# Attention and mixture of experts on one core: scores as three products of split q and k, the parts made by GpSimd

## The reference

```python
scores = scale * np.matmul(q, k.transpose(0, 1, 3, 2))
scores = np.where(mask, scores + bias[None], -1000000000.0)   # mask: 0 <= row - key < 128
attn = softmax(scores)
x = matmul(attn, v)                                            # (2304, 512)
expert = argmax(x @ w_gate); gate = its softmax probability
h = np.maximum(disp[e] @ w1[e], 0); y = h @ w2[e]               # disp: the rows of expert e, up to capacity
out[row] = gate * y[row]
```

## Time and profile before

| | |
|---|---|
| median of 3 runs | 436.08 us (435.88 to 436.37) |
| profiled execution | 436.13 us |
| its span, first to last instruction | 434.4 us |
| mean granted TensorE clock | 0.993 of full speed |
| TensorE matmul busy | 418.4 us (96%), 2860 instructions |
| VectorE busy | 276.9 us (64%) |
| ScalarE busy | 217.9 us (50%) |
| GpSimd busy | 100.0 us (23%) |

### The profile page before, as it was taken

The page is one execution under the profiler, slowest core; times in us unless marked ns, Lnnn a source line. Parts: engine busy times, 40 slices in busy tenths (PEclk is TensorE's granted clock), DMA queues, the critical chain, the costliest instruction groups (busy, mean ns, idle before and its releaser), DMA issues.

```text
span 434.4 us, 11059 instructions
## 1 busy us (share of the span) xinstructions
PE 418.4 (96%) x2860; PEld 341.3 (79%) x2861; DVE 276.9 (64%) x829; ACT 217.9 (50%) x576; POOL 100.0 (23%) x154
## 2 busy tenths in 40 slices
PE   6999999999999999899999999999999999999982
PEld 5778788787878877688888888888888888888871
DVE  4887788798988967865656627634657676233220
ACT  3878787787877743455544405515444445111100
POOL 5092066001301202412222211222222111222201
PEclk9999999999999999999999999999999999999997
DMA  9999399269621111465666605641676652111100
GB/s 175 238 272 197 81 285 222 80 212 246 152 74 50 51 39 24 154 230 192 204 237 223 230 27 166 212 148 61 212 238 207 208 193 94 48 48 38 45 27 16
DMA packets 78861, 63.59 MB, mean 146 GB/s; under 512 B 61614, under 2 KB 61614, under 8 KB 78832
## 3 DMA queue, kind: packets, MB, share of 16 engines
q1 hardware_dynamic: 71504, 51.66, 42.7%
q0 software_dynamic: 3520, 10.76, 7.6%
q10 hardware_dynamic: 3808, 0.80, 1.1%
HBM read 53.77 MB, written 10.23 MB: 147 GB/s over the span
## 4 chain that ended last, share of the span: by engine, by line
PE 90%; DVE 6%; issue 1%; DMA 1%; ACT 0%; POOL 0%; DVEq 0%; POOLq 0%; SPq 0%
PE ps L1282 52%; PE ps L1158 8%; PE ps L1126 7%; PE ps L1139 6%; PE ps L1170 5%; PE ps L1104 4%; PE ps L1302 4%; PE ps L1275 2%; DVE probs L760 1%; DMA q_rows<-in_q 1%; DVE weights_sb L1029 1%; DVE kT L772 1%; DVE sums_eps L778 0%; PE ps L1194 0%; DVE probsT L325 0%
## 5 line engine op out<-in xcount | busy, mean ns | idle before, releaser
L1282 PE MATMUL ps<-weights_sb,rowsT_hi 128*128 (+1 forms) x336 | 107.8, 402 | 1.3 <-DVE rowsT_lo L1016 1.3
L1282 PE MATMUL ps<-weights_sb,hiddenT_hi 128*128 x320 | 98.7, 389 | 1.2 <-DVE hiddenT_lo L1009 1.2
L698 ACT ACTIVATE hidden<-ps 128x512 f32<-128x512 f32 x20 | 11.9, 598 | 141.9 <-PE ps L1282 141.9
L1029 DVE TENSOR_TENSOR weights_sb<-raw,weights_sb 128x1024 f32 (+1 forms) x56 | 67.2, 1221 | 15.5 <-issue 10.0
L602 ACT ACTIVATE probs<-probs,mins 128x256 f32<-128x256 f32 (+2 forms) x160 | 73.8, 467 | 0.0
L1282 PEld LDWEIGHTS ps<-weights_sb,rowsT_hi 128*128 128x128 f32 x336 | 61.1, 188 | 15.2 <-issue 1.9
L1282 PEld LDWEIGHTS ps<-weights_sb,hiddenT_hi 128*128 128x128 f32 x320 | 60.0, 188 | 14.1 <-issue 1.4
L1282 PE MATMUL ps<-weights_sb,rowsT_lo 128*128 (+1 forms) x168 | 66.2, 394 | 0.0
L1009 DVE TENSOR_TENSOR hiddenT_lo<-ps,hiddenT_hi 128x512 fp32r<-128x512 f32 x40 | 25.8, 686 | 58.1 <-ACT hiddenT_hi L702 58.1
L1282 PE MATMUL ps<-weights_sb,hiddenT_lo 128*128 x160 | 62.4, 390 | 0.0
L687 ACT ACTIVATE weights_sb<-raw 128x1024 f32 (+1 forms) x56 | 56.6, 1068 | 0.0
(11 more groups left out here) (152 smaller groups left out, 535.6 us busy)
## 6 DMA issues: line engine op xcount, KB each, us to landing
raw<-in_moe_w SPq DMA_DIRECT2D x64, 512.0 KB, 4.4
q_rows<-in_q SPq DMA_DIRECT2D x16, 256.0 KB, 5.8
v_rows<-in_v SPq DMA_DIRECT2D x16, 256.0 KB, 4.5
x_rows<-x_sb SPq DMA_DIRECT2D x16, 256.0 KB, 4.6
k_rows<-in_k SPq DMA_DIRECT2D x13, 256.0 KB, 5.5
k_rows<-in_k ACTq DMA_DIRECT2D x3, 256.0 KB, 5.7
q_rows<-in_q SPq DMA_DIRECT2D x4, 128.0 KB, 3.9
k_rows<-in_k SPq DMA_DIRECT2D x4, 128.0 KB, 4.3
```

What stands on the lines that cost most here:

```text
L1029: vec.tensor_tensor(weights_sb[:, slot, 2 * layer + 1, part].rearrange("p s n -> p (s n)"), raw[:, j, :], weights_sb[:, slot, 2 * layer, p ...
L1282: ins = te.matmul(dst, left[a], right[c], start=first and n == 0, stop=last and n == 2)
```

## The change

ScalarE and VectorE write turned q and k no longer to `qT` and `kT` but back over the tile's own places in `q_rows` and `k_rows`, in float32. GpSimd makes of them the parts `qT` (hi and lo, two tiles deep), `kT_hi` and `kT_lo` in float32r: for q one copy and one subtraction of 512 elements, for k one copy of 512 and four subtractions of 128, for each of the tiles 2 to 19, and k alone for tile 1. The pieces of the first expert's weights, the one-hot columns and the first gather are put between them. The scores of tiles 0 and 1 of batch 0 are made whole in float32 from `q_rows` and `k_rows` (`score_whole`); the other 36 steps make three float32r products, hi x hi, hi x lo, lo x hi, for each head. SP's loads of the next batch wait for the parts in place of k_turned. TensorE's waits that protect the bank of the turning go to the new counters q_copied and k_copied. The buffers are placed so that the parts fit; `score_whole(0)` to `score_whole(3)` replace the first four scores.

```diff
-        qT, at = sb_at("qT", [P, TI, DC, P], at)
+        qT = []
+        for part in ("hi", "lo"):
+            tile, at = sb_at(f"qT_{part}", [P, 2, DC, P], at, F32R)
+            qT.append(tile)
...
-        kT, at = sb_at("kT", [P, DC, S], at)
+        kT_lo = []
+        kT_hi, at = sb_at("kT_hi", [P, DC, S], at, F32R)
...
             def load_next_qk(i, b):
 
-                sp.wait_ge(k_turned, (b - 1) * TI + i + 1)
+                if b == 1 and i < 2:
+                    sp.wait_ge(scored, 8)
+                sp.wait_ge(qT_ready, (b - 1) * TI + i + 1)
                 load_q(i, b)
+                sp.wait_ge(kT_ready, (b - 1) * TI + i + 1)
                 load_k(i, b)
...
+            def split_q(b, i):
+
+                n = b * TI + i
+                pool.wait_ge(q_copied, n + 1)
+                if n >= 4:
+                    pool.wait_ge(scored, 4 * (n - 1))
+                hi = qT[0][:, n % 2, :, 0:rows[i]]
+                link(g.tensor_copy(hi, q_turned_rows(i)))
+                g.tensor_tensor(qT[1][:, n % 2, :, 0:rows[i]], q_turned_rows(i), hi.bitcast(F32),
+                                ALU.subtract).then_inc(qT_ready, 1)
+
+            def split_k(b, i):
+
+                n = b * TI + i
+                pool.wait_ge(k_copied, n + 1)
+                hi = kT_hi[:, :, P * i:P * i + rows[i]]
+                link(g.tensor_copy(hi, k_turned_rows(i)))
+                for c in range(DC):
+                    last = g.tensor_tensor(kT_lo[c][:, P * i:P * i + rows[i]], k_turned_rows(i)[:, c, :],
+                                           hi[:, c, :].bitcast(F32), ALU.subtract)
+                last.then_inc(kT_ready, 1)
...
+            def batch(b):
+
+                for i in range(TI):
+                    n = b * TI + i
+                    if b == 0 and i < 2:
+                        if i == 1:
+                            split_k(b, i)
+                        continue
+                    split_q(b, i)
+                    split_k(b, i)
+                    if 3 <= n < 3 + CHUNKS:
+                        split_first_weights(0, n - 3)
+                    if TI + 3 <= n < TI + 3 + CHUNKS:
+                        split_first_weights(1, n - TI - 3)
+                    if n in (EARLY - 1, EARLY):
+                        half = (GROUPS[0][1] - GROUPS[0][0]) // 2
+                        lo = GROUPS[0][0] + half * (n - EARLY + 1)
+                        place_in_columns(0, lo, lo + half)
+                    if n == EARLY + 3:
...
+                        g.indirect_dma_start(first_rows[:, :], None, x_rows[0:(B - 2) * S, :],
...
-                nc.scalar.activation(qT[:, i, :, 0:rows[i]],
-                                     bank.rearrange("p (c s) -> p c s", c=DC)[:, :, 0:rows[i]],
-                                     ACT.Copy, scale=-(DH ** -0.5)).then_inc(qT_ready, 1)
+                nc.scalar.activation(q_turned_rows(i), bank.rearrange("p (c s) -> p c s", c=DC)[:, :, 0:rows[i]],
+                                     ACT.Copy, scale=-(DH ** -0.5)).then_inc(q_copied, 1)
...
-                vec.tensor_copy(kT[:, :, P * i:P * i + rows[i]],
-                                    bank.rearrange("p (c s) -> p c s", c=DC)[:, :, 0:rows[i]]).then_inc(kT_ready, 1)
+                vec.tensor_copy(k_turned_rows(i),
+                                bank.rearrange("p (c s) -> p c s", c=DC)[:, :, 0:rows[i]]).then_inc(k_copied, 1)
...
-                wait_alone(pe, qT_ready, b * TI + i + 1)
-                wait_for_rows(i, kT_ready, b * TI + i + 1)
-                for n in range(2):
+                n = b * TI + i
+                pe.wait_ge(qT_ready, n + 1)
+                pe.wait_ge(kT_ready, n + 1)
+                for m in range(2):
+                    for product, (a, c) in enumerate(((0, 0), (0, 1), (1, 0))):
+                        for odd in range(2):
+                            h = head(quad, 2 * odd + m)
+                            part = slice(DH * odd, DH * odd + DH)
+                            window = slice(first_key[i], first_key[i] + keys[i])
+                            right = kT_lo[h // 2][part, window] if c else kT_hi[part, h // 2, window]
+                            ins = te.matmul(scores_ps(kk % 2, odd)[0:rows[i], 256 * m:256 * m + keys[i]],
+                                            qT[a][part, n % 2, h // 2, 0:rows[i]], right,
+                                            start=(product == 0), stop=(product == 2))
+                            if m == 1 and product == 2:
+                                ins.then_inc(scored, 1)
...
-                        pe.wait_ge(kT_ready, tb * TI + ti)
+                        pe.wait_ge(k_copied, tb * TI + ti)
                         turn_q(tb, ti)
                     if turns and quad == 1:
-                        pe.wait_ge(qT_ready, tb * TI + ti + 1)
+                        pe.wait_ge(q_copied, tb * TI + ti + 1)
                         turn_k(tb, ti)
```

More of the change, by code:

```diff
@@ L199, in attention_moe @@
         mixT, at = sb_at("mixT", [P, 2, P], at)
+        tile, at = sb_at("kT_lo0", [P, S], at, F32R)
+        kT_lo.append(tile)
         at = start = max(at, weights_end)
@@ L212, in attention_moe @@
         in_column, at = sb_at("in_column", [P, UNITS, COLS], at, FP16)
+        for c in (1, 2):
+            tile, at = sb_at(f"kT_lo{c}", [P, S], at, F32R)
+            kT_lo.append(tile)
         hidden = []
@@ L235, in attention_moe @@
         k_turned = sem("k_turned")
+        q_copied = sem("q_copied")
+        k_copied = sem("k_copied")
         qT_ready = sem("qT_ready")
@@ L515, in place_in_columns @@
                                     ALU.is_equal).then_inc(onehots_ready, 1)
[L517 to L523, removed]
+            def batch(b):
[16 more added lines that the diff above has]
+                    if n == EARLY + 3:
+                        pool.wait_ge(first_src_ready, 1)
+                        pool.wait_ge(rows_stored, TI + GROUPS[0][1])
+                        pool.wait_ge(gates_stored, 2 * (B - 2) * 16)
+                        g.indirect_dma_start(first_rows[:, :], None, x_rows[0:(B - 2) * S, :],
+                                             bass.IndirectOffsetOnAxis(ap=first_src_i[:, 0:1], axis=0)
+                                             ).then_inc(first_landed, 16)
+            pool.sem_inc(qT_ready, 2)
+            pool.sem_inc(kT_ready, 1)
+            pool.wait_ge(consts_done, CONSTS)
+            for b in range(B):
+                batch(b)
             place_in_columns(1, *GROUPS[1])
@@ L1119, in score, with score_whole @@
                 i, quad = divmod(kk, 2)
[L1120 to L1122 removed]
+                n = b * TI + i
[13 more added lines that the diff above has]
+                                ins.then_inc(scored, 1)
+            def score_whole(kk):
+                i, quad = divmod(kk, 2)
+                pe.wait_ge(q_copied, i + 1)
+                pe.wait_ge(k_copied, i + 1)
+                for m in range(2):
                     for odd in range(2):
[L1124 removed]
+                        h = head(quad, 2 * odd + m)
                         part = slice(DH * odd, DH * odd + DH)
[L1126 to L1129 removed]
+                        ins = te.matmul(scores_ps(kk % 2, odd)[0:rows[i], 256 * m:256 * m + keys[i]],
+                                        q_rows[part, i, P * (h // 2):P * (h // 2) + rows[i]],
+                                        k_rows[part, 0:i + 1, P * (h // 2):P * (h // 2) + P],
+                                        start=True, stop=True)
+                        if m == 1:
                             ins.then_inc(scored, 1)
@@ L1241, in batch @@
                             pe.wait_ge(back_kept, b * STEPS + kk - 1)
-                        score(b + (kk + 2) // STEPS, (kk + 2) % STEPS)
+                        if first and kk < 2:
+                            score_whole(kk + 2)
+                        else:
+                            score(b + (kk + 2) // STEPS, (kk + 2) % STEPS)
                     if last and kk == 2:
```

33 lines of the change are left out of this document (15 added, 18 removed).

## The result

The changed kernel takes 439.81 us (median of 9 executions, 437.74 to 442.98) against 436.08 (9 executions, 435.87 to 436.48): a ratio of 1.0094, 95% interval 1.0069 to 1.0119 (ratios here and below are of the means, times are medians). It is slower by 3.7 us, where the forecast was 0.8. The profiled execution took 439.72 us, its span 437.8: 1.9 us lie around it, 1.7 before. The executions line up by their mean granted clock: 437.74 us at 0.995, 439.21 to 439.81 at 0.990 and 0.991, 440.78 to 441.25 at 0.986 and 0.987, 442.98 at 0.984.

A forecast was written before the change was run, and what follows sets the result against it. TensorE was taken to bound attention, VectorE next. Terms: -3.3 scores, +0.6 GpSimd, +0.6 adds, -0.3 won back, +2.7 search and ranks, +0.5 VectorE later more often: +0.8 on 436.08, forecast 436.9 us, range 433.4 to 440.5.

The forecast's parts named there:

- The case forecast: Attention: faster scores, but VectorE stands behind GpSimd in the search and eats the gain; 436.9 us, chance 0.53.
- B: Rival: GpSimd becomes the bound, its parts late at scores in the two runs of weight pieces; 439.8 us, chance 0.10.
- E: Rival: a score pair costs 0.143 us, so three products save nothing and the costs remain; 440.2 us, chance 0.04.
- Part 1: TensorE's score groups: 0.90, 0.68, 0.88 us for 256, 192, 128 keys; 3.3 us saved, bounds 1.2 to 6.0.
- C: Rival: score windows under 512 columns do not run as a single pass; 451.8 us, chance 0.05.
- D: Rival: the halves of a single-pass score pair run one after the other; about 456 us, chance 0.03.
- Part 2: GpSimd's new parts: 4.3 us a tile, 7.7 with weights, against 8.0; 1.2 us margin at tile 12's score; 0.6 us lost.
- Part 3: VectorE standing behind GpSimd: 0.6 us lost at adds, 0.3 won back, 2.7 lost in search and ranks, bounds 0 and 5.
- A: Rival: the saving stays, as only instructions like the add stand or GpSimd is idle during the search; 434.0 us, chance 0.25.
- the 0.6 us for the adds: VectorE's small scalar add on the sums, once a tile: mean wait 0.3 us, 18 times, covered except where VectorE is busiest.
- Part 4: SP's loads, row stores, one-hot columns, first gather and renamed waits: moved or delayed at no cost.
- the 1.95 us stand: VectorE's scalar add at 23.46 us in the kernel before, held by a GpSimd subtract; 0.3 us forecast won back.

The follow-up runs named there:

- e1: The changed kernel, but GpSimd begins the q parts of tile 3 of batches 2 and 3 only after VectorE's top-expert search: 435.28 us, ratio 0.9975.
- e9: The changed kernel with GpSimd's q subtraction cut into four pieces of 128 columns: 436.24 us, ratio 0.9999.
- e7: The changed kernel with VectorE's top-expert search moved from step 1 to the ends of steps 0 and 2: 435.31 us, ratio 0.9974.
- e3: The changed kernel with hi parts written by VectorE and ScalarE, lo parts zero, no GpSimd parts after tile 1: 434.06 us, 0.9942 of the kernel before.
- e2: The changed kernel with all GpSimd work, but each score one whole float32 product of the hi parts: 442.39 us, ratio 1.0129.
- e4: The kernel before with two extra sums in VectorE's queue at the search of batches 2 and 3, plus an added array: 442.89 us, ratio 1.0147.
- e5: The changed kernel with 14 extra transposes ahead of TensorE's wait in step 2 of batch 2: 440.03 us, ratio 1.0076.
- e6: The kernel before with one unused array of four bytes a partition declared ahead of the others: 434.07 us, ratio 0.9944.
- e8: The changed kernel with the search spread over steps 0 and 2, whole tile 0 scores in batches 1 to 3, no 1e-9 add: ten of twelve executions 435.96 to 437.21 us.

## Why the prediction was right or wrong

The case forecast, a gain eaten up by VectorE standing behind GpSimd, is what happened, and e1 shows it; the time was 2.9 us too low. 439.81 lies outside that case's own range (435.3 to 438.5) and within 433.4 to 440.5 only because that range took in rivals B and E. Both are met by chance: B's mechanism, parts late at the score, is absent (0.17 us more than before at each of two scores), and E's pair of 0.143 us takes 0.12.

**Part 1, right.** 0.91, 0.68 and 0.81 us for 0.90, 0.68 and 0.88. Only the case of 128 keys was off, and not by its pairs: they come every 0.11 us, as forecast, but 0.15 us is left beside six of them, not 0.21. Counted up, 22 x 0.16 + 8 x 0.12 - 6 x 0.17 = 3.5 us for 3.3. The measured pitch of 0.12 us stands against the 109 ns estimated from the Trainium skill ("TensorE: Matmul & The Clock Gate", "Back-to-back issue gap"). C and D are false too.

**Part 2, right.** Subtractions of 1.28 and 0.46 us, copies of 0.61 (92.67 to 93.28), for 1.25, 0.40 to 0.45 and 0.61; lost at the scores some 0.3 us for 0.6. e9 confirms the margin: 0.4 us more a tile opens it.

**Part 3, right for the search, wrong for the adds.** I took a stand of up to 0.4, mean 0.3 us, for the add of 1e-9 (L842), beside the parts of k. Its mean stand is 0.19 us, and the sign, over 0.3 us on most tiles, is not met (9 of 20). But twice the add fell beside a 512-wide subtraction of q and took 0.83 us, once just ahead of the search. In the search the stand is 0.37 + 1.08 = 1.45 us in batch 2 (forecast 1.4) and 0.25 + 1.13 = 1.38 in batch 3 (forecast 1.0; just as many parts fall on it there). No wait shows at the ranks, where I had 0.3. Together 2.8 us for 2.7, of which, by e1, 2.43 - 1.09 and 2.43 - 1.18 = 2.6 us reach TensorE. A stand ends within 0.1 us of the GpSimd instruction beside it, whatever its length (e1, e7, e9), which is the rule cited from the Trainium skill, "SBUF — State Buffer", "Who interferes with whom"; the traces agree for instructions with both inputs in SBUF, and A is false. Two with one tensor input in SBUF stand as well: the add, and L931 (in_tile, 1.02 us for 0.30 at 114.69, beside a subtraction of q from 114.39 to 115.66).

**The terms that failed** are the 0.6 us for the adds and the 0.5 us for "VectorE, as TensorE gets shorter, is the later one more often": 1.1 us forecast, 2.2 measured. In e1, free of the stand in the search, 1.09 - 0.21 = 0.88 and 1.18 - 0.21 - 0.24 = 0.73 us are still lost behind it, 0.3 at 117 us, and 0.3 in two waits that grew, at 109 and 149 us. e3, where GpSimd makes no parts, loses 0.26 and 0.31 us behind the search and the same 0.3 at the two waits, so 0.9 us is VectorE's own, for 0.5. The other 1.3 us, by this difference, are stands of small instructions: the add ahead of the search (0.67 and 0.29 us), and L931 ahead of the wait at 117. I had spread the adds evenly over the tiles and called them covered. The times of batch 2 say the same: the score starts 1.14 us earlier than before (92.87 for 94.01), the search only 0.47 (92.49 for 92.96), and the 0.67 between the two is the add's stand; in e3 it is 0.76 and 0.60. And of the 0.2 us of margin at the copy of the probabilities 0.15 is the way from the end of a copy to the mix (95.85 to 96.00), so less than 0.1 was free.

**What was not in the sum** is the clock: 1.5 - 0.3 + 0.16 (the gain of one score) = 1.4 us from mix 22 to mix 23 for its one fall in the profiled execution, while the executions spread over 5 us. The one at a mean clock of 0.995 took 437.74 us, 0.8 above the forecast, so most of the miss at the median comes with the clock. I had priced the stand as time, not as an idle TensorE.

Together -3.5 (part 1) + 0.3 (scores that wait for parts) - 0.4 (the 1.95 us stand) + 2.6 (search) + 2.2 + 1.4 (clock) = +2.6 of the lag of 2.7; the first score was 0.6 us late as well in this execution (8.25 for 7.63 us), which differs from one execution to the next. **Part 4, right:** no load, store or gather is waited for.

## What to carry to other kernels

A gain on the bounding engine spends the margins of the others, so read the margin at a critical hand-over after the gain has been subtracted, not from the kernel before, and take off the way from the copy's end to its reader. When work is moved to GpSimd, list the VectorE instructions that read SBUF alone, small scalar ones included, in the whole step ahead of a copy TensorE waits for, and set the longest GpSimd instruction beside each: a mean over all tiles hides the two that count. Then hold GpSimd back there, cut its instructions short, or move VectorE's work to a step with room, and check that the cut does not make GpSimd late. A cost and its cover can be told apart in two runs, the cost without the gain and the gain without the cost.

## What the runs showed of the hardware that was not expected

- The clock falls from 2.4 to 1.2 GHz for 3.4 us behind some of TensorE's waits of 1.96 to 2.91 us (the changed kernel, e2, e4, e5, e6, e8). Behind others of 1.96 to 3.21 us (137 us in the changed kernel, 141 and 191 in e4) it does not, and in the attention of e1, e7, e8 and e9, with waits of up to 1.76 us, it never does. A fall costs 1.4 to 1.6 us in the attention. The kernel before is not free of it: of its 41 executions beside e1 to e8 three took 438.44 to 439.06 us, at a mean clock of 0.989 and 0.990.
- Four bytes more ahead of the arrays, with the same instructions, make a tile of the experts 12.25 instead of 12.35 us, 2.0 us in all. An experiment that adds an array should have a twin with the array alone.
- VectorE's bias instruction (L824), with one input in PSUM and one in SBUF, kept its 0.42 us while GpSimd subtracted beside it from 91.02 to 92.73:

```profile
91.81 0.42 DVE L824 CUSTOM_DVE_ANT_0 probs<-ps,bias 128x256 f32<-128x256 f32 x1
```
